# A sine of one zero column ahead of ScalarE's first copy, and a wait that moves from the channel layer's first product to the first turning of x2

## The reference

```python
# retention: chunks of 128 tokens, 12 in all
state = gamma * state + k_t v_t^T ;  x_t = scale * q_t state
# wave layer
theta = x @ w_theta                       # 512 x 512
zr, zi = x * cos(theta), x * sin(theta)
u = x + w_tok_r @ zr + w_tok_i @ zi       # mixing over the 768 tokens
x2 = u + relu(u @ w_ch)                   # channel layer, 512 x 512
# two small perceptrons, over tokens (256 wide) and over channels (1536 wide)
u2 = x2 + (relu(x2^T @ w_tok1) @ w_tok2)^T
out = u2 + relu(u2 @ w_ch1) @ w_ch2
```

## Time and profile before

| | |
|---|---|
| median of 3 runs | 449.81 us (449.34 to 450.46) |
| the profiled execution: its own time | 449.38 us |
| its span on the core | 447.6 us (the time has 1.8 us around it) |
| PE busy, PEld busy | 437.8 us (98%), 382.3 us (85%) |
| DVE, ACT, POOL busy | 210.4, 127.9, 99.1 us |
| mean granted clock of TensorE | 1.0 of full speed |

### The profile page before, as it was taken

How to read it: one execution, slowest core, us unless ns; L and a number is a source line. 1 busy time by engine, 2 the same in 40 slices (tenths; PEclk the granted TensorE clock), 3 DMA queues, 4 the chain that set the end, 5 groups by cost and what they waited for, 6 DMA issues and landing times.

```text
span 447.6 us, 6232 instructions
## 1 busy us (share of the span) xinstructions
PE 437.8 (98%) x2676; PEld 382.3 (85%) x2676; DVE 210.4 (47%) x304; ACT 127.9 (29%) x194; POOL 99.1 (22%) x80
## 2 busy tenths in 40 slices
PE   7799999999999999999999999999999999999996
PEld 4587878899999999999889888888888888888885
DVE  3789998799999993244335211112211113111113
ACT  0455654734455456012313211111111110111110
POOL 2422241000200009940998940000000000000000
PEclk9999999999999999999999999999999999999999
DMA  8955697540784111030241000000200001000002
GB/s 309 395 218 202 267 235 168 105 142 0 183 182 154 47 49 48 13 129 1 94 142 47 1 0 1 0 0 12 84 1 0 0 1 73 21 1 0 1 0 94
DMA packets 9980, 38.29 MB, mean 86 GB/s; under 512 B 993, under 2 KB 2145, under 8 KB 8161
## 3 DMA queue, kind: packets, MB, share of 16 engines
q1 hardware_dynamic: 7856, 28.31, 17.3%
q0 software_dynamic: 1952, 9.44, 9.2%
q10 hardware_dynamic: 144, 0.14, 0.1%
HBM read 34.75 MB, written 3.15 MB: 85 GB/s over the span
## 4 chain that ended last, share of the span: by engine, by line
PE 95%; DVE 2%; DMA 1%; ACT 1%; issue 0%; DVEq 0%; ACTq 0%
PE ps L780 85%; PE ps L797 3%; PE ps L837 3%; PE ps L851 2%; PE ps L927 1%; PE ps L811 1%; PE ps L827 1%; DMA qkv_in<-qkv 1%; DVE w_sq L578 1%; DVE res L774 1%; DVE prob L594 1%; ACT L477 0%; ACT w_sq L460 0%; ACT x_hi L477 0%; DVE res L613 0%
## 5 line engine op out<-in xcount | busy, mean ns | idle before, releaser
L780 PE MATMUL ps<-u,w_a 128*128 128x512 f32 x432 | 103.3, 389 | 0.0
L768 DVE SCALAR_TENSOR_TENSOR w_sq<-ps,w_sq 128x512 fp32r<-128x512 f32 x36 | 24.9, 692 | 156.7 <-ACT w_sq L561 156.7
L780 PEld LDWEIGHTS ps<-u,w_a 128*128 128x128 f32 x432 | 81.1, 188 | 16.8
L780 PE MATMUL ps<-tw,zs 128*128 128x384 f32 x504 | 88.1, 334 | 0.0
L780 PEld LDWEIGHTS ps<-tw,zs 128*128 128x128 f32 x504 | 87.3, 188 | 0.1
L561 ACT ACTIVATE w_sq<-ps 128x512 fp32r<-128x512 f32 x36 | 21.6, 599 | 168.0 <-PE ps L780 168.0
L780 PE MATMUL ps<-w_sq,ch_a 128*128 128x512 f32 x216 | 51.9, 389 | 0.0
L780 PE MATMUL ps<-w_sq,w_b 128*128 128x512 f32 x216 | 51.4, 389 | 0.0
L780 PEld LDWEIGHTS ps<-w_sq,w_b 128*128 128x128 f32 x216 | 40.5, 188 | 8.4
L780 PEld LDWEIGHTS ps<-w_sq,ch_a 128*128 128x128 f32 x216 | 40.5, 188 | 8.4
L780 PE MATMUL ps<-ut,w_sq 128*128 128x384 f32 x192 | 35.6, 339 | 0.7 <-issue 0.7
(11 more groups left out here) (83 smaller groups left out, 473.1 us busy)
## 6 DMA issues: line engine op xcount, KB each, us to landing
qkv_in<-qkv SPq DMA_DIRECT2D x11, 1024.0 KB, 6.1
stage<-weights SPq DMA_DIRECT2D x17, 512.0 KB, 3.3
raw<-tok POOLq DMA_DIRECT2D x7, 1152.0 KB, 8.9
cols_out<-res SPq DMA_DIRECT2D x12, 256.0 KB, 2.1
raw<-tok SPq DMA_DIRECT2D x6, 384.0 KB, 8.1
raw<-tok POOLq DMA_DIRECT2D x3, 384.0 KB, 9.2
qkv_in<-qkv SPq DMA_DIRECT2D x2, 512.0 KB, 5.0
raw<-theta_w SPq DMA_DIRECT2D x2, 512.0 KB, 8.6
```

The source lines that it names most:

```text
L768: dve.scalar_tensor_tensor(out=h2[:, f % 2, 1, :], in0=bank(BK_H2 + f % 4), scalar=0.0, in1=f32(h2[:, f % 2, 0, :]), op0=ALU.max, op1=ALU. ...
L780: mm = pe.matmul(dst, left(l), right(r), start=first and n == 0, stop=last and n == 2, skip_group_check=True)
```

## The change

A tile `spare` of one column is added. ScalarE, behind the issue of its transfer and ahead of the wait for it, waits for `idle_ready` and takes the sine of one column of the zeroed tile `idle` into `spare`, which nothing reads. And the wait for `y_kept` at 28 stands no longer in `channels(0)` but in `turn_x2(0)`, behind its wait for `x2_kept`.

```diff
         cst = sb("cst", [P, N_CONST])
+        spare = sb("spare", [P, 1])
...
             act.dma_start(cst[:, 0:C_OUT], consts[:, 0:C_OUT]).then_inc(const_in, 16)
+
+            act.wait_ge(idle_ready, 1)
+            act.activation(spare[:, :], idle[:, 0:1], ACT.Sin)
             act.wait_ge(const_in, 16)
...
                 half, b, n = q // (B * NK), q // NK % B, q % NK
                 if q == 0:
                     split_done(pe, P_T12 - 1)
-                    pe.wait_ge(y_kept, STEPS)
                 if q >= 2:
                     pe.wait_ge(x2_kept, q - 1)
...
             def turn_x2(n):
                 b, c = turned(n)
                 pe.wait_ge(x2_kept, (n // 3 + 1) * NK)
+                if n == 0:
+                    pe.wait_ge(y_kept, STEPS)
                 if n >= 3:
                     pe.wait_ge(x2_lo, n - 2)
```

## The result

The changed kernel takes 446.26 us in the median of 5 runs (445.87 to 447.63), the kernel before 449.81 (449.34 to 450.65): a ratio of 0.9918, 95% interval 0.9902 to 0.9935.

The account below looks back on a forecast made before the run. TensorE, busy for 98% of the span at its upper clock, was taken as the bound. 1.76 + 0.86 = 2.62 us off the profiled 449.38 gave 446.8, plus 0.43 to the median: 447.2 us, range 446.5 to 448.7.

Parts of the forecast that it names:

- GpSimd's turn: In theta(0): GpSimd's k_dec slips between the two theta_low on VectorE, so the second took 2.067 us against 1.227.
- One load, early, and free: On ScalarE at the start: one table load, over by about 4 us at no cost; x_hi starts 1.29 us earlier.
- The load's delay and GpSimd's turn: From x_hi to scores(2): without the load, k_dec no longer precedes the second theta_low; scores(2) starts 1.76 us earlier.
- Enough slack behind it: Behind scores(2): no new wait of TensorE, smallest slack 0.5 us; the second load's removal is worth nothing.
- The second edit: Channel layer's first product: without the wait for y_kept it starts 0.86 us earlier, bounds 0.69 and 0.86.
- the two edits' terms: Start and channel layer together: 1.76 us from the early load plus 0.86 from the moved wait, 2.62 us.
- the last one of the sum: Whole execution: the 0.43 us between median and profiled execution was added to 446.8, giving 447.2 us.
- the rival for slower: With no pause before the channel layer, TensorE's clock falls to its lower level for a stretch; 452.5 us; chance 0.04.
- the first edit: ScalarE's start: the early table load brings scores(2) forward by 1.76 us, bounds 1.07 and 1.8.

## Why the prediction was right in its mechanisms and wrong in its size

The starts that the traces show, side by side (us; the time is that of the profiled execution):

| kernel | scores(0) takes | outputs(0) starts | first theta_low starts | second takes | theta(0) from its first product to scores(2) in the chain | time |
|---|---|---|---|---|---|---|
| before, first profile | 2.10 | 8.85 | 14.53 | 2.07 | 3.54 (GpSimd's turn) | 449.38 |
| before, again | 1.58 | 8.41 | 14.10 | 2.07 | 4.73 (clock 0.64) | 450.16 |
| before, first pause filled | 1.16 | 7.93 | 13.62 | 1.22 | 3.01 | 447.96 |
| changed, first profile | 1.16 | 8.02 (takes 1.98, clock) | 14.03 | 2.06 | 3.55 (GpSimd's turn) | 447.63 |
| changed, again | 1.55 | 8.19 | 12.80 | 1.22 | 2.97 | 445.73 |
| changed, first pause filled | 2.08 | 8.75 | 13.27 | 1.22 | 3.00 | 446.21 |

Executions with a lowered clock, over all runs:

| kernel | lowered | of |
|---|---|---|
| before | 54 | 90 |
| before, wait moved | 9 | 12 |
| before, GpSimd held back | 8 | 12 |
| before, first pause filled | 6 | 12 |
| before, both pauses filled | 0 | 11 |
| sine or copy alone | 3 | 13 |
| changed | 2 | 11 |
| changed, first pause filled (two versions) | 0 | 11 |
| changed, with a delay (two versions) | 2 | 13 |

Point by point:

- **One load, early, and free.** Right: at 1.16 to 2.44, the sine 0.20 us. The copy starts 1.29 us earlier against `finish_x(0)`, as the earlier trace rows had it. The Trainium skill (ScalarE: Activation LUTs, section What ACT_TABLE_LOAD costs) gives 2.66 us for a switch; the trace agrees with the 1.28 us of load in it and, with 1.29 us in all, not with the drain beside the load.
- **The load's delay and GpSimd's turn.** Right in size, counted from the start of `outputs(0)`: 1.74 us against 1.76 forecast. The Trainium skill (SBUF — State Buffer, section SBUF: two separate sides) has a GpSimd instruction and a VectorE instruction with two SBUF inputs exclude each other. With `k_dec` held back all four instructions took their short times, which agrees; that they exclude each other whole, and don't share, rests on the end times in the earlier trace rows.
- **Enough slack behind it.** Right: in the good executions nothing new waits between 18 and 40 us; the second load was worth nothing.
- **The second edit.** 0.94 us by the traces, 1.0 us by the medians of one group of runs, 0.86 forecast.
- **Like against like.** The first profile (449.38) and that of the changed kernel with the first pause filled (446.21) have the same slow `scores(0)` and no fall of the clock. They are 3.17 us apart: 0.10 in the start, 1.80 to `scores(2)`, 0.98 from there to the last additions, 0.3 behind them. So the two edits' terms, 2.62 in the sum, measured 2.78, and the last stores add 0.3. That would have put the forecast at about 446.75, inside the range.
- **The step that failed** is the last one of the sum: "The median of the runs shown, 449.81, lies 0.43 above the profiled one", carried over to the changed kernel as a constant. Behind it stands the reading of the clock under what bounds the kernel, "its granted clock stands at the upper of its two levels, 2.4 GHz, in all 40 slices", so that a fall of the clock entered only as the rival for slower. That was true of the profiled execution and not of the kernel. In 54 of 90 executions of the kernel before the clock is lowered (median 450.08, against 448.21 for the other 36), so its median lies among these, above the profiled one. With the early load and nothing else added it is 5 of 24, and the changed kernel's median, 446.26, lies within 0.05 us of the like execution without a fall (446.21). That is some 0.4 us of the 0.94 us by which 447.2 was missed. The second thing put at nothing was the end of the program, the 0.3 us of the last stores.
- **What the medians of the first edit hold.** 2.6 us for the sine alone is a difference of mixtures. Executions with the full clock alone give 448.11 for the kernel before and 446.78 for sine and copy alone, 1.3 us; those with a lowered clock 450.06 and 447.90 (three only), 2.2 us. The rest is that fewer executions are lowered.

The fast groups: the kernel before with its first pause filled (447.96) has neither GpSimd's turn nor a fall of the clock, the changed one again took 445.73. The 2.23 us between them look like 1.29 of load plus 0.94, but that is luck: `outputs(0)` started 0.26 earlier in the kernel before, the last stores took 0.3 longer there, and the two nearly cancel.

What stays open: why `scores(0)` takes 1.16 us in one execution and 2.10 in the next of otherwise equal programs. Its pace points at the clock: the four warming products of 512 columns in front of it took 3.5 to 3.8 us, 0.9 us each, and the two like them that were added behind it 1.13, 0.56 us each. But the granted clock reads 1.00 from 5 to 8 us in every trace, so this is inferred and not shown. Open too is why a fall came in some executions with a given pause and not in others: in the four traces with the slow `scores(0)` there is none, behind pauses of up to 1.99 us. In traces of kernels whose pauses were not filled the fall lay in `theta(0)` twice and at 8 to 12 us twice; where it lay in the executions without a trace isn't known. That the early load makes falls rarer is shown by the counts (5 of 24 against 54 of 90), and that filled pauses take them away by 0 of 11 against 11 of 23. That the load does it by lengthening the pause is argued from these and from two traces with a fall right behind that pause; the delay in the load's place, 1 of 7, doesn't bear it out.

## What to carry to other kernels

Ask of a pause of TensorE near the start not only how long it is but what the clock does in the products behind it, and take a second profile before calling the clock steady: a median that lies well above the profiled execution can be the sign that the kernel has more than one course, and the mean clock of each execution sorts them. Compare profiles of like starts down to the last store before adding up terms: a new tile or instruction can change something far from its place. A table load belongs ahead of ScalarE's first wait; an activation of one column, a sine or a copy here, puts it there. Where a wait guards data that the next products don't touch, move it to the first instruction that reads them; at this place it was worth 0.25 us more than the idle time that the trace showed.

## What the runs showed of the hardware that I had not expected

TensorE's clock fell to its lower level for most of some 4 us behind pauses of 1.5 to 2.0 us in the first 20 us of the program, in some executions of one and the same program: 0.57 over 8 to 12 us behind a pause of 1.53, 0.64 over 15.5 to 20.2 us behind one of 1.98. In both, TensorE had been busy for some 5 us in front of the pause (1.46 to 6.49 and 8.41 to 13.49). From 21 to 440 us the granted clock was 1.00 in all thirteen traces compared here. Filling both pauses with products on a zero tile brought the executions with a lowered clock from 11 of 23 to 0 of 11. The last four stores of 256 KB landed in 2.1 us in the median in every kernel with the early activation and its tile, and in 2.3 in every one without.
